# Moving the routing chain, the table scatters and the first token gathers between two stages of a fused attention and expert kernel

## The reference

```python
ret = (scale * q @ k.T) * decay          # attention with a decay mask, 4 x 8 heads, 576 x 64
x   = ret @ v                            # -> 2304 x 512
xn  = x / rms(x) * rms_g                 # dense layer, 512 -> 1536 -> 512
y   = (silu(xn @ w_gate) * (xn @ w_val)) @ w_out
e   = argmax(y @ moe2_w_gate)            # expert layer, 8 experts, one per token
out = softmax(y @ moe2_w_gate)[e] * sigmoid(y @ w_output_gate)[e] * (relu(y @ w1[e]) @ w2[e])
```

## Time and profile before

| | |
|---|---|
| median of 3 runs | 831.35 us (829.65 to 832.52) |
| profiled execution | 832.47 us, its span 830.8 us |
| PE busy | 785.0 us, 94% |
| DVE, ACT, POOL busy | 456.4, 431.2, 438.7 us |
| dense layer ends, routed layer begins | 530.8, 556.9 us |

### The profile page before, as it was taken

The page is one execution under the profiler, slowest core; times in us unless marked ns, Lnnn a source line. Parts: engine busy times, 40 slices in busy tenths (PEclk is TensorE's granted clock), DMA queues, the critical chain, the costliest instruction groups (busy, mean ns, idle before and its releaser), DMA issues.

```text
span 830.8 us, 15029 instructions
## 1 busy us (share of the span) xinstructions
PE 785.0 (94%) x5029; PEld 692.7 (83%) x5029; DVE 456.4 (55%) x806; ACT 431.2 (52%) x845; POOL 438.7 (53%) x437
## 2 busy tenths in 40 slices
PE   6998899999999999999999999739999999999995
PEld 5887798997889998788999877528888888888884
DVE  3489775674647667453776436115545455545452
ACT  2566655564665555565655434204545445535543
POOL 2579986796758789674788326840112111221221
PEclk9999999999999999999999999959999999999998
DMA  9984342122202242220223022534455554564552
GB/s 306 320 276 155 120 161 75 52 90 73 67 27 77 67 141 85 77 64 26 77 77 127 26 63 72 108 91 140 131 176 171 162 174 157 164 194 148 163 179 94
DMA packets 48939, 102.88 MB, mean 124 GB/s; under 512 B 7553, under 2 KB 8835, under 8 KB 48486
## 3 DMA queue, kind: packets, MB, share of 16 engines
q1 hardware_dynamic: 43510, 90.61, 34.4%
q0 software_dynamic: 4944, 10.96, 4.3%
q10 hardware_dynamic: 432, 0.63, 0.2%
HBM read 92.71 MB, written 10.40 MB: 124 GB/s over the span
## 4 chain that ended last, share of the span: by engine, by line
PE 82%; POOL 8%; issue 3%; DMA 3%; DVE 1%; ACT 1%; SPq 0%; POOLq 0%; DVEq 0%; ACTq 0%
PE banks L1591 10%; PE banks L1593 9%; PE banks L1592 9%; PE banks L1817 5%; PE banks L1819 5%; PE banks L1818 5%; PE banks L1653 5%; PE banks L1655 5%; PE banks L1654 5%; PE banks L1575 5%; PE banks L1577 5%; PE banks L1576 5%; POOL AL L540 2%; PE banks L1687 1%; POOL slot_table L619 1%
## 5 line engine op out<-in xcount | busy, mean ns | idle before, releaser
L1591 PE MATMUL banks<-BH,AH 128*128 128x384 f32 x504 | 170.5, 338 | 3.7 <-ACT p_m L1260 2.6
L1593 PE MATMUL banks<-BH,AL 128*128 128x384 f32 x504 | 168.5, 334 | 0.0
L1592 PE MATMUL banks<-BL,AH 128*128 128x384 f32 x504 | 168.5, 334 | 0.0
L1591 PEld LDWEIGHTS banks<-BH,AH 128*128 128x128 f32 x504 | 94.6, 188 | 10.9 <-issue 5.0
L540 POOL TENSOR_TENSOR AL<-s_ab,AH 128x1024 fp32r<-128x1024 f32 x36 | 88.6, 2462 | 25.2 <-ACT AH L1214 25.2
L1592 PEld LDWEIGHTS banks<-BL,AH 128*128 128x128 f32 x504 | 94.6, 188 | 0.1
L1593 PEld LDWEIGHTS banks<-BH,AL 128*128 128x128 f32 x504 | 94.6, 188 | 0.0
L1653 PE MATMUL banks<-dH,hidH 128*128 128x512 f32 x216 | 85.7, 397 | 3.3 <-POOL dL L554 2.3
L673 POOL DMA_INDIRECT out<-yo,rec_cur x24 | 23.1, 962 | 118.2 <-ACT yo L1446 115.7
L554 POOL TENSOR_TENSOR dL<-wraw,dH 128x256 fp32r<-128x256 f32 x72 | 59.6, 849 | 49.0 <-ACT dH L1230 48.7
L1654 PE MATMUL banks<-dL,hidH 128*128 128x512 f32 x216 | 84.4, 391 | 0.0
(11 more groups left out here) (194 smaller groups left out, 1654.4 us busy)
## 6 DMA issues: line engine op xcount, KB each, us to landing
wraw<-w_moe SPq DMA_DIRECT2D x168, 256.0 KB, 2.7
wraw<-w_moe SPq DMA_DIRECT2D x36, 512.0 KB, 3.5
vr<-v_rows SPq DMA_DIRECT2D x15, 320.0 KB, 4.7
qt<-q_t SPq DMA_DIRECT2D x16, 288.0 KB, 5.3
y_rows<-y_sb SPq DMA_DIRECT2D x6, 768.0 KB
kt<-k_t SPq DMA_DIRECT2D x15, 288.0 KB, 4.2
kr<-k_rows SPq DMA_DIRECT2D x16, 256.0 KB, 3.2
hid<-w_out_t SPq DMA_DIRECT2D x3, 1024.0 KB, 8.5
```

The lines of the kernel that those rows point to most:

```text
L1591: mm(to, wh, bh, start=first and k == 0, stop=False, skip_group_check=True)
L1592: mm(to, wh, bl, start=False, stop=False, skip_group_check=True)
L1593: i = mm(to, wl, bh, start=False, stop=k == 1, skip_group_check=True)
```

## The change

- DVE: `choose` moves from (2, 0) to (1, 1), `own_gate` from (2, 1) to (2, 0), `ranks` from (5, 0) to (3, 1), `slot_rows` from (5, 1) to (4, 0), and every later piece up by one group. PE: `count_tiles` behind group 3, `match_ids` behind group 8. ACT: `exps` in step 3. POOL: `gates` in step 5.
- POOL: no scatter between low halves any more. Ten scatters behind the last low half, then the three first gathers, then the other eight scatters, the wait for all scatters, the table loads, and the second block's gathers.
- The last 384 rows: PE signals each of the three tiles when it is finished (`s_tile`), ACT and DVE copy each one then, and SP stores each one by itself (256 KB).
- `WARM` from 6 to 10.

```diff
-WARM = 6
+WARM = 10
@@ SP
-                for a in range(2):
+                for a in range(1 if blk == BLOCKS - 1 else 2):
...
-                    if blk * 2 + a == 2 * BLOCKS - 1:
-                        sp.wait_ge(s_ylast, 2)
...
             store_y(BLOCKS - 1)
+            for j in range(TPH):
+                t = TILES - TPH + j
+                if j == 0:
+                    sp.wait_ge(s_y, TILES - 2)
+                else:
+                    sp.wait_ge(s_ylast, j)
+                sp.dma_start(y_rows[t * P:(t + 1) * P, :], y_sb[:, t, :]).then_inc(s_ystore, 16)
@@ POOL
-            AT_F = {7: range(0, 3), 8: range(3, 6), 9: range(6, 9)}
-            AFTER = range(9, TILES)
+            EARLY = TILES // 2 + 1
...
-                    if last and f == 6:
+                    if last and f == 5:
                         gates()
                         pool.wait_ge(s_pad, 32)
-                    if last and f in AT_F:
-                        scatter_records(AT_F[f])
-            scatter_records(AFTER)
+            scatter_records(range(EARLY))
...
-            pool.wait_ge(s_scat, 16 * TILES)
-            load_record(row)
-            pool.dma_start(rec_cur[:], table[0:SLOTS, :].rearrange("(p g) c -> p g c", g=GROUPS)).then_inc(s_rec0, 16)
             pool.wait_ge(s_ids, 1)
-            pool.wait_ge(s_ystore, 16 * 2 * BLOCKS)
+            pool.wait_ge(s_ystore, 16 * (2 * BLOCKS - 1 + TPH))
             for g in range(GROUPS):
                 pool.indirect_dma_start(
...
             pool.sem_inc(s_issued, 1)
+            scatter_records(range(EARLY, TILES))
+            pool.wait_ge(s_scat, 16 * TILES)
+            load_record(row)
+            pool.dma_start(rec_cur[:], table[0:SLOTS, :].rearrange("(p g) c -> p g c", g=GROUPS)).then_inc(s_rec0, 16)
             gather(0)
@@ DVE
-            dve.wait_ge(s_down, BLOCKS * 2 * F1)
             for j in (1, 2):
+                dve.wait_ge(s_tile, j + 1)
                 V.tensor_copy(y_sb[:, TILES - TPH + j, :], banks[:, DOWN[1][j], :]).then_inc(s_ylast, 1)
@@ ACT
-            act.wait_ge(s_down, BLOCKS * 2 * F1)
+            act.wait_ge(s_tile, 1)
             S.activation(y_sb[:, TILES - TPH, :], banks[:, DOWN[1][0], :], ACT.Copy).then_inc(s_y, 1)
@@ PE
-                i.then_inc(s_down, 1)
+                    if n == N1 - 1 and a == 1:
+                        i.then_inc(s_tile, 1)
+                if not (n == N1 - 1 and a == 1):
+                    i.then_inc(s_down, 1)
```

More of the change, by code:

```diff
@@ L259, in build @@
         s_wt, s_vp, s_v4, s_vt, s_V = sem("s_wt"), sem("s_vp"), sem("s_v4"), sem("s_vt"), sem("s_V")
-        s_lgp, s_lg4, s_lgt, s_lgs = sem("s_lgp"), sem("s_lg4"), sem("s_lgt"), sem("s_lgs")
+        s_tile, s_lgp, s_lg4, s_lgt, s_lgs = sem("s_tile"), sem("s_lgp"), sem("s_lg4"), sem("s_lgt"), sem("s_lgs")
         s_rt, s_below, s_ogate, s_exp, s_onehot, s_cnt, s_slot, s_plan = (
@@ L1030, in route_step @@
             def route_step(f, half):
+                if (f, half) == (1, 1):
+                    choose()
                 if (f, half) == (2, 0):
-                    choose()
-                if (f, half) == (2, 1):
                     own_gate()
+                if (f, half) == (3, 1):
+                    ranks()
+                if (f, half) == (4, 0):
+                    slot_rows()
                 if (f, half) == (5, 0):
-                    ranks()
+                    slot_columns()
                 if (f, half) == (5, 1):
-                    slot_rows()
+                    slot_match(0)
                 if (f, half) == (6, 0):
-                    slot_columns()
+                    slot_match(1)
                 if (f, half) == (6, 1):
-                    slot_match(0)
+                    slot_match(2)
                 if (f, half) == (7, 0):
-                    slot_match(1)
+                    plan_counts()
                 if (f, half) == (7, 1):
[L1047 to L1050, removed]
                     plan_rows()
-                if (f, half) == (10, 0):
+                if (f, half) == (9, 0):
                     find_ids()
@@ L1352, in down_step @@
                     high_b(blk + 1, DOWN_B[f])
-                if blk == BLOCKS - 1 and f == 4:
+                if blk == BLOCKS - 1 and f == 3:
                     exps()
@@ L1755, in _ @@
                         turn_logits(blk)
-                    if blk == BLOCKS - 1 and n == n0 + 4:
+                    if blk == BLOCKS - 1 and n == n0 + 3:
                         count_tiles()
-                    if blk == BLOCKS - 1 and n == n0 + 9:
+                    if blk == BLOCKS - 1 and n == n0 + 8:
                         match_ids()
```

## The result

The changed kernel takes 827.07 us (median, 826.09 to 827.07); the kernel before, run beside it, 831.46 (829.65 to 832.52). The ratio is 0.9947 with a 95% interval of 0.9934 to 0.9959: 4.4 us faster (3.4 to 5.5), where I had forecast 8.9. The time lies outside my range of 818.3 to 825.6.

The account below looks back on a forecast made before the run. Bound: TensorE's matmuls in order (82% of the chain), with PE idle 14.23 us between stages behind POOL's scatters and gathers. First gather 8.9 us earlier, other terms nothing: 831.35 - 8.9 = 822.4 us, range 818.3 to 825.6.

Parts of the forecast that it names:

- Part 1: Routing chain one to two groups earlier: first stall stays, second goes, down projection ends at 529.6, 1.2 us earlier.
- Part 2: POOL issues ten scatters, then the gathers: tenth scatter ended at 537.0, first gather possible at 537.3.
- Part 3: Last rows stored tile by tile: stores of y arrive last by a little, first gather starts at 538.1.
- the stores are confirmed only behind the scatters: Rival: gathers effectively wait for the tenth scatter to land, first gather 540.7, gain 6.3, 825.1 us; chance 0.10.
- the rule of the Trainium skill: For the stores: a completion increment lands only after every earlier write of that DMA engine, across its queues.
- the 2.0 us and 436 GB/s of the Trainium skill: Stores of y in at about 535, gathers bound by POOL at 537.3, 0.8 us more gain than forecast.
- Part 4: Behind the first gather all moves 8.9 us earlier; eight late scatters and second block's gathers, 10 us cover, cost nothing.
- Part 5: Ten warm-up products before the transposes: delay nothing; value for TensorE's clock taken as nothing, bounds nothing to 2.9 us.
- the clock is kept: Rival: TensorE's clock stays up through the shorter idle stretches around the transposes, 2.9 us more, 819.5 us; chance 0.33.
- The sum: Whole kernel: 8.9 us off the median of 831.35, giving 822.4 us.

Follow-up runs that it names:

- e7: Changed kernel with POOL's old order: scatters between low halves and behind the last, then the wait and loads, first gathers last; 829.23 us.
- e4: Changed kernel with six of the ten early scatters back between low halves, four behind the last low half, eight behind the gathers; 822.45 us.
- e8: e6 with half of the gate sums one POOL step earlier, seven scatters between low halves, four behind the last, seven behind the gathers; 818.61 us.
- e1: Changed kernel with all 18 scatters behind the first gathers; 834.62 us.
- e9: e4 with no scatter behind the last low half: six between low halves, twelve behind the gathers; 821.40 us.
- e10: e8 with no scatter behind the last low half: seven between low halves, eleven behind the gathers; 817.80 us.
- e5: e4 without the last eight scatters, so eight tiles' output rows are left out; 821.37 us.
- e3: Changed kernel with six warm-up products again instead of ten; 827.30 us.
- e6: e4 with twelve warm-up products, and two, two and one more behind the transposes of the three token groups; 819.72 us.
- e2: Changed kernel with one 768 KB store of the last rows in place of three small ones; 826.70 us.

## Why the prediction was wrong

**Part 1** was right in each number, once the 2.03 us by which this execution is early are taken off. One stall of 1.45 us, one group earlier, was worked out for 511.82, that is 509.79; it stands at 509.78. The last low half ended at 522.22 (worked out: 524.25, that is 522.22). The down projection lost its second stall and was 1.2 us shorter, as forecast. e7 adds that the second stall goes with the scatters, not with the chain (nine of them between low halves; the six of e4, in steps 7 and 8, bring no wait); e8, that the first one is the gate sums'.

**Part 2** was right: POOL was through with ten scatters at 535.06, and the gather could have started at 535.36 (worked out: 537.3, that is 535.27).

**Part 3 is the step that failed.** The first gather was to be 8.5 us behind the last down matmul and was 12.97 (10.2 to 13.0 over the kernels with the same ten scatters). I had taken "the old 7.9 us of data" from the earlier trace rows as the stores' own cost, and had set the landing where that data would end. Three things are wrong in this.
- Those 7.9 us were themselves lengthened by the scatters that were in flight before: alone, the same data took 4.1 us and the stores landed 5.35 us after the first issue. By luck it was about right for the data in after (8.2 us).
- The end of the data was not the landing. In after 3.2 us lie between them, 0.3 in e1. This is the largest part of the miss of 4.5 us.
- The last small store was issued 3.0 us behind W (530.55 in the chain), not 1.3. The data ended 8.8 us behind W, where my gather at 538.1 left it 7.7; that is another 1.1 us of the miss.

The rival "the stores are confirmed only behind the scatters" was nearest: e1, e9 and e10 show that scatters in flight hold the stores up. That a store is confirmed behind the last scatter is not shown to the letter, since in after it was confirmed at 539.63 and the scatters' last landing record is at 540.26. I gave it 0.10 and reckoned its first gather to 11.1 us behind the last down matmul, still 1.9 less than came, because it let the tenth scatter land 3.9 us after its start. In after it landed 6.2 us after (534.09 to 540.26), as it too ran beside the stores. I had taken the rule of the Trainium skill as speaking for this rival and still gave it a fifth of the forecast's chance, with "no row separates the two" as the only reason; the lack of a row was a reason for an even split. The other rule that I used there, the 2.0 us and 436 GB/s of the Trainium skill (page "DMA: Bandwidth & Descriptors", section "Anatomy of one DMA"), is stated for DMAs that GpSimd issues, which the prediction didn't say.

**Part 4** was right in that the second block's gathers are hidden: the record load came at 557.70 and the gathers at 560.38, some 20 us ahead of their reader. "It costs nothing" was wrong for the eight late scatters, since I looked for their cost only at the gathers queued behind them. ACT, whose queue holds no scatter, was late for its first h2H, and the routed stage took 1.1 us more. e5 shows that it isn't late without the late scatters; e9, on time with twelve of them, shows that they alone don't decide it, and how they do it stays open.

**Part 5** had the right value, in after by luck: the clock fell at 541.6 and rose at about 555, and the four products were worth nothing (e3), but ahead of the transposes PE was idle for 7.61 us and not for the 2.9 that the argument was about. e4 and e9 test it. In e4 the clock fell at 539.5, within 2.34 us of idle time, before any transpose; in e9 it fell at 543.0 after two of the bursts. One reading was off as well: by the earlier trace rows the three bursts fill 3.0 us (1.01 each), not 1.5; at the upper clock they fill 1.8 (0.60 each in e6). The rival "the clock is kept" fell in after and came true in e6, once the idle time between the bursts was filled.

**The sum.** -1.2 - 7.7 had been forecast. The stages give -1.2 - 3.2 + 1.1 = -3.3; with the middle one of the three hold-ups (11.4 behind W, -4.8) they give -4.9. The median of -4.4 lies between the two. The 2.0 us ahead of group 3 are in neither, so that the agreement with the median is in part chance. The range failed as well: its upper end was the rival's 825.1 and half a microsecond, with no room for a hold-up longer than the rival's, nor for any cost behind the gathers.

## What to carry to other kernels

A transfer's time read from a trace belongs to what else was in flight: before reusing such a number as a cost, look for the same bytes with nothing beside them, and count to the landing, not to the last byte. Small scattered writes that nobody waits for soon are best put where no store or fetch with a waiting reader overlaps them; here, in the queue's idle stretches between low halves (e4; e7, which puts scatters behind step 6 too, made PE wait twice). When work is moved off a queue's critical stretch, look at the engines beside its new place too, not only at the instructions behind it in its own queue.

## What the runs showed of the hardware

- 1.57 MB of row stores in two to four DMAs landed 5.35 us after the first issue with nothing else in flight (5.35, 5.35, 5.34 in e1, e9, e10), 8.8 and 8.0 beside weight loads (the blocks of 296.12 and 439.78 in before), 7.1 to 7.7 with four scatters behind the last low half (e4, e5, e6, e8), and 9.6 to 12.3 with nine to twelve (e2, e7, before, e3, after). Their 2 KB packets took 0.084 us on average in e1 and 0.163 in after. What it is in a scatter (18 of them, 128 rows each, a small record a row) that does this was not tried.
- Stores without data in flight could still be unconfirmed for 3 us, while scatters were landing.
- ACT stood still for 11.28 us in e1, from 553.46 until 564.74, 0.66 us behind the last landing record of a scatter (564.08), and for about 2 us in after, with "remote" as the only releaser named. In e5, without late scatters, it didn't. A slow 8 KB code fetch (2.25 to 2.68 us in after, e2, e3, e4, e6 and e8; 1.57 in e10, 1.77 in e1; 0.31 to 0.67 in before, e5, e7 and e9) goes with it in some runs. The cause stays open.
- A 16 KB code fetch took 2.4 to 3.4 us beside scatters and stores (after, e2 to e6). It took 1.1 and 1.3 with no scatter in flight (e1, e9), but also 1.4 and 1.0 in e7 and e8, and 2.25 and 2.68 in e10 and before. Where it was slow and SP had stores to issue (after, e2 to e6), one issue ended 0.3 to 0.5 us behind it.
- In e9 the transposes followed the warm-up after 0.58 us of idle time, with 1.91 and 1.84 us between the bursts of four, and the granted clock still fell to the lower level at 543.0 (in e4, with 2.34 us of idle time ahead of the first burst, at 539.5); with two products behind each burst (e6, e8, e10) it stayed at the upper one. That was worth about 1.8 us in e6.
